# Attention and two expert layers on one core: the products with the values for two groups in every second group

## The reference

```python
scores = scale * np.matmul(q, k.transpose(0, 1, 3, 2))
mask = (rel >= 0) & (rel < window)
scores = np.where(mask, scores, -1000000000.0)
scores = scores - np.max(scores, axis=-1, keepdims=True)
attn = np.exp(scores)
attn = attn / (np.sum(attn, axis=-1, keepdims=True) + 1e-09)
return np.matmul(attn, v).astype(np.float32)
```

## Time and profile before

| | us |
|---|---|
| median of 3 runs | 1078.38 |
| lowest, highest | 1077.81, 1081.57 |
| the profiled execution | 1076.49 |
| its span (first to last instruction) | 1074.7 |
| TensorE busy in the span | 1062.6 |
| VectorE, ScalarE, GpSimd busy | 588.3, 327.8, 386.8 |

### The profile page before, as it was taken

One profiled execution on the slowest core, in us unless ns is written; L12 is line 12 of the kernel. 1 busy time (PEld: TensorE's weight loads), 2 busy tenths in 40 slices (PEclk: granted clock), 3 DMA queues, 4 the chain that ended last, 5 costly groups with the idle time before them and its releaser, 6 DMA issues.

```text
span 1074.7 us, 20097 instructions
## 1 busy us (share of the span) xinstructions
PE 1062.6 (99%) x6053; PEld 931.9 (87%) x6054; DVE 588.3 (55%) x1226; ACT 327.8 (31%) x724; POOL 386.8 (36%) x358
## 2 busy tenths in 40 slices
PE   8999999999999999999999999999999999999998
PEld 7878999999999999999988888888888888888886
DVE  6887434363363463453447775565555556555554
ACT  7987122342342432432352111020302021110222
POOL 4667990030030030120185415070706143250486
PEclk9999999999999999999999999999999999999999
DMA  7985525411311311211074536172616344331676
GB/s 218 276 264 190 176 89 187 127 59 30 118 59 30 117 59 30 98 59 30 26 250 153 161 80 174 39 207 46 195 47 161 85 117 127 82 104 39 168 242 235
DMA packets 199634, 133.18 MB, mean 124 GB/s; under 512 B 128752, under 2 KB 161408, under 8 KB 199584
## 3 DMA queue, kind: packets, MB, share of 16 engines
q1 hardware_dynamic: 177728, 75.14, 25.9%
q10 hardware_dynamic: 16032, 38.47, 10.9%
q0 software_dynamic: 5824, 18.95, 5.1%
HBM read 85.87 MB, written 42.73 MB: 120 GB/s over the span
## 4 chain that ended last, share of the span: by engine, by line
PE 93%; POOL 2%; DMA 2%; issue 1%; DVE 1%; SPq 0%; POOLq 0%; ACT 0%; DVEq 0%
PE bank L873 28%; PE bank L1041 20%; PE bank L1062 20%; PE bank L905 14%; PE bank L1075 3%; PE bank L817 2%; PE bank L844 2%; PE bank L827 1%; POOL token_rows_a L750 1%; PE bank L811 1%; DMA token_rows_b<-expert_rows,slots_u 1%; PE bank L958 1%; DMA q_sb<-in_qT 1%; POOL token_rows_a L763 1%; DMA k_sb<-in_kT 0%
## 5 line engine op out<-in xcount | busy, mean ns | idle before, releaser
L873 PE MATMUL bank<-x_parts,mlp_weights 128*128 128x384 f32 x1704 | 309.4, 336 | 0.0
L873 PEld LDWEIGHTS bank<-x_parts,mlp_weights 128*128 128x128 f32 x1704 | 298.3, 188 | 5.3
L1041 PE MATMUL bank<-expert_parts,xT_high 128*128 (+1 forms) x688 | 216.6, 396 | 0.0
L1062 PE MATMUL bank<-expert_parts,hT_high 128*128 (+1 forms) x688 | 212.2, 390 | 0.0
L732 POOL TENSOR_TENSOR expert_parts<-raw_expert_a,expert_parts 128x512 fp32r<-128x512 f32 x64 | 81.4, 1305 | 234.3 <-ACT expert_parts L1372 232.0
L905 PE MATMUL bank<-mlp_weights,hidden_parts 128*128 128x512 f32 x648 | 162.1, 395 | 0.0
L1062 PEld LDWEIGHTS bank<-expert_parts,hT_high 128*128 128x128 f32 x688 | 129.0, 188 | 26.9 <-issue 0.4
L1041 PEld LDWEIGHTS bank<-expert_parts,xT_high 128*128 128x128 f32 x688 | 125.8, 188 | 24.3 <-issue 0.4
L905 PEld LDWEIGHTS bank<-mlp_weights,hidden_parts 128*128 128x128 f32 x648 | 120.2, 188 | 23.4 <-issue 1.0
L1041 PE MATMUL bank<-expert_parts,xT_low 128*128 (+1 forms) x344 | 134.4, 391 | 0.0
L1062 PE MATMUL bank<-expert_parts,hT_low 128*128 (+1 forms) x344 | 134.2, 390 | 0.0
(11 more groups left out here) (220 smaller groups left out, 1230.1 us busy)
## 6 DMA issues: line engine op xcount, KB each, us to landing
raw_expert_a<-in_w ACTq DMA_DIRECT2D x32, 512.0 KB, 4.6
raw_expert_b<-in_w ACTq DMA_DIRECT2D x32, 512.0 KB, 4.2
x_row<-routed_rows SPq DMA_DIRECT2D x172, 64.0 KB, 2.6
expert_rows<-y_row SPq DMA_DIRECT2D x43, 256.0 KB, 2.0
expert_rows<-zeros SPq DMA_DIRECT2D x4, 2304.0 KB, 11.9
v_sb<-in_v SPq DMA_DIRECT2D x32, 256.0 KB, 3.9
q_sb<-in_qT SPq DMA_DIRECT2D x15, 288.0 KB, 3.7
k_sb<-in_kT SPq DMA_DIRECT2D x15, 288.0 KB, 4.1
```

The lines of the kernel that those rows point to most:

```text
L873: last = nc.tensor.matmul(bank[:, 0:CHUNK], w_sb[:, i, wp, at:at + P], xp[:, par, part, k, :], start=n == 0, stop=n == 3 * KB - 1)
L1041: last = nc.tensor.matmul(ps[half][:, 0:512], (xTh, xTl)[xp][:, buf, k, :], ew_sb[:, bass.ds(slot, 1), wp, k * F2 + half * 512:k * F2 + ha ...
L1062: last = nc.tensor.matmul(y_bank(t)[:, 0:D], (hTh, hTl)[hp][:, f, :], ew_sb[:, bass.ds(slot, 1), 2 + wp, f * D:(f + 1) * D].rearrange("p a ...
```

## The change

`pT_sb` gets three places instead of two, and moves out of attention's area to memory that holds a block of weights later on. TensorE does no value products in even steps; in odd steps it does those of two groups, G - 5 and G - 4, one after the other, behind the transposes. ScalarE's copy of pT waits for the value products three groups back instead of two. VectorE copies two groups out in even steps (G - 6 and G - 5), none in odd ones; one copy more stands behind the last step.

```diff
-    pT_sb = att.take("pT_sb", [P, 2, GROUP, P], F32)
...
+    pT_sb = at("pT_sb", [P, 3, GROUP, P], F32, W_OFF + UNDER_BLOCK * 2 * COLS * 4 + KB * CHUNK * 4)
...
         TO_T, TO_PV = 3, 4
+        assert U % 2 == 0
...
-                                            v_sb[:, par, odd, w0 // P, hs], pT_sb[:, u % 2, a, hs],
+                                            v_sb[:, par, odd, w0 // P, hs], pT_sb[:, u % 3, a, hs],
...
                     if not first or u >= TO_T:
                         pe_transpose(pe, G - TO_T, (u - TO_T) % U)
-                    if not first or u >= TO_PV:
-                        pe_pv(pe, G - TO_PV, m if u >= TO_PV else m - 1, (u - TO_PV) % U)
+                    if u % 2 == 1 and (not first or u > TO_PV):
+                        for back in (TO_PV + 1, TO_PV):
+                            pe_pv(pe, G - back, m if u >= back else m - 1, (u - back) % U)
...
             act.wait_ge(pT_done, G + 1)
-            if not (isinstance(G, int) and G < 2):
+            if not (isinstance(G, int) and G < 3):
-                act.wait_ge(pv_done, G - 1)
+                act.wait_ge(pv_done, G - 2)
-            nc.scalar.copy(pT_sb[:, u % 2], ...
+            nc.scalar.copy(pT_sb[:, u % 3], ...
...
                     dve_max(dve, G, u)
-                    if not first or u >= TO_PV + 1:
-                        back = u - TO_PV - 1
-                        copy_out(dve, G - TO_PV - 1, back % U, m if back >= 0 else m - 1)
+                    if u % 2 == 0 and not first:
+                        for back in (TO_PV + 2, TO_PV + 1):
+                            copy_out(dve, G - back, (u - back) % U, m if u >= back else m - 1)
...
             last = LOOPS * U - 1
+            copy_out(dve, last - TO_PV - 1, U - 2 - TO_PV, LOOPS - 1)
             dve_sums(dve, last, U - 1)
```

More of the change, by code:

```diff
@@ L191, in attention_moe_kernel @@
     UNDER_BLOCK = X_BLOCK - 2
+    pT_sb = at("pT_sb", [P, 3, GROUP, P], F32, W_OFF + UNDER_BLOCK * 2 * COLS * 4 + KB * CHUNK * 4)
+    assert KB * CHUNK + 3 * GROUP * P <= 2 * COLS
     xh_first = at("x_high_first", [P, KB, CHUNK], F32R, W_OFF + UNDER_BLOCK * 2 * COLS * 4)
@@ L1227, in act_copy_pT @@
             act.wait_ge(pT_done, G + 1)
-            if not (isinstance(G, int) and G < 2):
-                act.wait_ge(pv_done, G - 1)
-            nc.scalar.copy(pT_sb[:, u % 2], ps[2 + u % 2][:, 0:GROUP * P].rearrange("p (a b) -> p a b", a=GROUP)
+            if not (isinstance(G, int) and G < 3):
+                act.wait_ge(pv_done, G - 2)
+            nc.scalar.copy(pT_sb[:, u % 3], ps[2 + u % 2][:, 0:GROUP * P].rearrange("p (a b) -> p a b", a=GROUP)
                            ).then_inc(pT_copied, 1)
```

## The result

| | before | after |
|---|---|---|
| median of 22 runs, us | 1078.36 (1077.23 to 1081.57) | 1080.12 (1078.82 to 1082.92) |
| the profiled execution, its span, us | 1076.49, 1074.7 | 1078.82, 1077.0 |

The ratio is 1.0016 with a 95% interval of 1.0009 to 1.0022: 1.8 us slower (1.0 to 2.4), which is less than the half per cent that the prediction took for no change, but clear of zero. The forecast was +0.8.

What follows compares the result with a forecast made beforehand. Attention was taken as bound by a ring through TensorE and ScalarE, with VectorE the bound in the root steps. Terms 0 + 0.2 + 0.3 + 0.3 = +0.8 us on the median of 1078.38 gave 1079.2 us, range 1075.6 to 1082.4.

Steps and rivals of the forecast that it cites:

- The ring: Attention's loop through TensorE and ScalarE's queries: 5.35 us an item before, 10.70 per two items before and after the change.
- Rival 1: TensorE's saving comes through in attention, items of 4.4 and 5.4 us by turns: -4.2 us, 1074.2 us; chance 0.13.
- Half one: Item starting at an even step, without value products in it: next item's mask product 5.00 us after its own.
- Half two: Item starting at an odd step, two value groups ahead of the next step's transposes: 5.70 us.
- plain rounds 0: Steps 6 to 17: TensorE's saving becomes a wait at the mask product and VectorE's second copy is covered: 0 us.
- the squares: Steps 18 to 25: VectorE's extra copy before a maximum delays the first sum on TensorE from 51.52 to 51.8: +0.3 us.
- shorter or equal: Root steps: TensorE's waits there for VectorE's copies would not grow, and cost nothing.
- root steps: Steps 26 to 31, bound by VectorE: six copies instead of five stand before its diagonals in step 30: +0.3 us.
- Scaling rounds: Steps 36 to 43: VectorE's second copy makes steps 0.20 and 0.19 late; with step 33 starting 0.20 sooner, +0.2 us.
- the far end: SyncE's key loads: none late at the median landing of 4.1 us, put at 0; a late landing or two, 0.8.
- Rival 2: Transposes wait 0.3 to 0.5 us for GpSimd's normalising in the five late rounds: 1081.6 us; chance 0.2.
- Rival 3: Half one isn't shortened, something other than ScalarE holding the mask product, while half two is 0.35 longer: +2.5, 1081.6 us; chance 0.07.

Runs made afterwards that it cites:

- before_q0: Kernel before, with the next item's queries scaled one step earlier on ScalarE and VectorE: ratio 1.0011 [0.9999, 1.0022].
- after_q0_keys: Changed kernel, with queries scaled one step earlier and the keys' load ahead of the queries' load: 1077.72 us, ratio 0.9991 to the kernel before.
- the second pair: The kernels before and after, both unchanged, profiled once more: 1077.49 and 1077.83 us, one execution each.
- early_open: Changed kernel, with pairs only in steps 5 to 17, queries a step earlier only there, keys' load first: 1075.41 us, ratio 0.9987 to the kernel before.
- even_pairs: Changed kernel, with the pairs of value products in even steps and VectorE's two copies in odd ones: 1082.89 us, ratio 1.0047 to the kernel before.
- same_before: Kernel before, unchanged, profiled once more: 1077.49 us, one execution.
- three_places: Kernel before, with only the three places of pT in their new memory, no pairs: 1078.12 us against 1077.88, ratio 1.0003.
- same_after: Changed kernel, unchanged, profiled once more: 1077.83 us, one execution.
- late_weights: Changed kernel, with the loads of the third weight block moved two items later: ratio 1.0010 [1.0001, 1.0018] to the kernel before.
- after_q0: Changed kernel, with the next item's queries scaled one step earlier on ScalarE and VectorE: ratio 1.0014 [1.0000, 1.0027] to the kernel before.
- after_keys: Changed kernel, with SyncE loading the next keys ahead of the next queries: ratio 1.0003 [0.9994, 1.0012] to the kernel before.

## Why the prediction was right, and where it was off

**The ring: right.** The forecast's main step was that TensorE's saving turns into waits for ScalarE's queries. They are there (4.6 us over ten waits), and opening the ring alone (before_q0) brought the plain stretch to TensorE's pace; with the ring and the key loads open (after_q0_keys) pairs were quicker there than no pairs. Rival 1 (4.4 and 5.4 by turns) did not happen, although its first half appeared once queries and keys were early. The Trainium skill (TensorEngine Tiling (Array Packing), Key Properties) says that changing the tiling mode drains TensorE. The trace agrees: the value products' weight loads sit idle 0.17 us behind nearly every run of transposes, 44 such times before and 18 (21 with those put down to VectorE's copy) after. But nothing of it reached the time.

**Half one: 0.17 too short.** I put 5.00 us and it measured 5.17, since I took 1.37 from the mask product to the copy where this item shows 1.44, and 0.81 from the queries to the mask product where it shows 0.91. The 1.44 is not the transposes' doing: ScalarE's last instruction for the step before starts at 26.84 and lasts 0.21, to 27.05, and the copy follows at 27.08. Half two was put at 5.70 and measured 5.67 to 5.74. The four items from step 6 took 5.19, 5.74, 5.17 and 5.67, together 21.77, where the ring as I summed it gives 21.40. The same stretch before was itself 0.18 above the ring's 21.40: its items took 5.42, 5.35, 5.49 and 5.32, of which the prediction had shown only the last, and it took 5.35 for all. So the term "plain rounds 0" measured +0.2, and +0.4 in the second pair, where step 18 waited 0.42 for keys.

**VectorE: right in the squares, and together.** From step 18 to the first sum took 14.44 us (36.48 to 50.92; 14.20 before), forecast 14.48. The whole stretch to step 32 rose by 0.51 and 0.50, the forecast was 0.3 + 0.3 less 0.2 for the earlier step 33, which lies just behind it: from 32 to 33 after took 1.51 (65.46 to 66.97) against 1.75 (65.79 to 67.54). One reading was wrong there: TensorE's waits for copies were to be "shorter or equal", and they grew from 1.1 us (L844) to 2.1 (L847), twice each. They stand in the root steps, where VectorE is the bound; that they cost nothing, as the prediction says, is argued and not shown. That the pairs make this stretch longer is shown (early_open has none there and takes the time of before); that it is by VectorE's two copies in a row rests on the forecast's walk and the numbers that fit it, since even_pairs, which was to test it, lost its time to late keys.

**Scaling rounds: the items but for one.** Steps 33, 36, 39, 42 start at 66.97, 72.67, 77.89 and 83.83: 5.70, 5.22 and 5.94, forecast 5.70, 5.19, 5.70. From step 42 to 45 it took 5.06, forecast 5.20.

**The keys: a far end that came, with and without the pairs.** I had costed the later value loads at 0, with 0.8 as the far end, by landing times taken from the trace before. That trace had the quickest landing of all for step 42: 4.0 us, where same_before had 5.1 and three_places 5.6, both without pairs; after had 5.1, same_after 5.6, late_weights 5.0. In after, the row of step 42 names ScalarE's queries as the last to come. They started at 82.78, which is 77.89 plus the 4.89 that the ring gives; but the product followed 1.05 later and not 0.81, and the keys, issued at 78.36, landed at 83.46, 0.37 ahead of it, much as in same_after (78.28 plus 5.6, product at 84.32). The item was 0.24 longer than the ring's 5.70 in one profile and 0.86 in the other; without pairs, step 42 waited for keys 0 (before), 0.37 (same_before) and 0.86 us (three_places). So no run shows that the pairs made these keys late. The 0 for the change may stand; what was too narrow was the reading of landings from a single trace.

**The sum, by stretches.** In the first pair of profiles the change cost +0.19 in the plain rounds, +0.24 to the first sum, +0.27 from there to step 32, -0.24 in step 32, +0.73 from step 33 to 42 and -0.12 from there to the gated layer: 1.07 from step 6, where the forecast had 0, 0.3, 0.3, -0.2 and +0.4 for the rest, 0.8. The second pair has 1.53, with more waiting for keys on the side of after.

**The fill** was not in the sum. Steps 4 and 5 without value products start sooner (11.47 for step 5 against 13.23 and 12.44), but step 6 starts at 14.71 and 14.43 against 15.74 and 15.15, and waits for keys in three of these four profiles; what comes through depends on a transfer. For this reason step 47 ended at 94.34, not near 95.

**The other signs**: 21 idle times for "issue" of 5.8 us in all (24 of 4 to 5 foretold); mask products 1.17 and 2.10 apart (1.15 and 2.11); waits for the queries of up to 0.6. Of the 5.8 us, 18 idle times of 0.17 make 3.1 and the two long ones 2.5. **Rival 2** (transposes wait for the normalising) was small: four waits, 0.9 us in all, the longest 0.3. **Rival 3** (half one not shortened) did not occur.

The profiles do not account for the +1.76 us of the medians. From step 6 on they give 1.07 and 1.53, but at the first low product the two pairs differ by only 0.04 and 0.81 us, since step 6 came earlier with the pairs. Over all profiles step 6 starts at 14.22 to 15.09 in kernels with pairs and at 14.24 to 15.74 in those without, so that part may be chance. The scatter in the expert layer is larger than any of these. That attention became longer from step 6 on, by about 1 us, is shown; the rest of the 1.8 us is not placed. The measured change is twice the forecast's 0.8, and the range (1075.6 to 1082.4) would have held no change as well, so that it was met says little; the waits and the items by turns say more.

## What to carry to other kernels

Work taken from the busiest engine is worth nothing while a ring through another engine sets the pace; add up the ring first, then open it, and only then lighten the engine, in those rounds where no third engine is the bound. The time of a transfer is a spread and not a number: one load at one place landed in 4.0, 5.1 and 5.6 us in three kernels whose loads stood alike. Hold the slack against that spread, from more than one profile, before a late transfer is put down to a change.

## What the runs showed of the hardware

The clock: in even_pairs TensorE waited 2.22 us for keys, and its next products ran at a granted clock of 0.57 on average over 4 us. The same happened once more there, from 64 to 68 us (0.59), and once each in after_q0 and after_q0_keys (0.64 and 0.57 from 64 to 68 us), each time behind pauses of TensorE (1.78 to 2.72 us busy in the 4 us before). A wait of 1.92 us in after_keys had no such cost, nor had before_q0 after 2.49 us busy from 60 to 64, nor the kernel after (2.48 us busy from 56 to 60). So a stall can cost nearly twice what its wait shows (2.2 and 1.6 us in even_pairs); what decides between them these runs do not tell.

The idle time of the value products' weight loads behind transposes was the same in both kernels: 0.17 us in 44 of 47 times before and in 18 of 21 after. The averages (0.19 and 0.28) differ only by the few long ones.

Landings of one 288 KB load of keys, the one for step 42, went from 4.0 to 5.6 us over the six profiles in which SyncE issues it behind the queries and the queries are scaled in the second step (before, same_before, three_places, after, same_after, late_weights), at a DMA share of 0.96 to 1.01 from 78 to 82 us.
